# Where the values times their bonus are made: ScalarE instead of GpSimd, in a kernel of three stages

## The reference

```
def _attn_ref(r, k, v, w, u):                    # (batch 2, heads 8, seq 768, dim 48)
    state = zeros((B, H, D, D))
    for t in range(S):
        kt, vt, rt = k[:, :, t], v[:, :, t], r[:, :, t]
        cur = einsum('bhd,bhe->bhde', u[None] * kt, vt)
        y[:, :, t] = einsum('bhd,bhde->bhe', rt, state + cur)
        state = w[None, :, :, None] * state + einsum('bhd,bhe->bhde', kt, vt)
...
attn_out -> x (2, 768, 384) -> _moe_ref (8 experts, 384 -> 1024 -> 384) -> _moe2_ref (384 -> 1024, spatial 768 x 768, 512 -> 384)
```

## Time and profile before

| | |
|---|---|
| median of 3 runs | 408.51 us (406.87 to 411.73) |
| the profiled execution | 408.09 us, of which 405.9 us span |
| busy, share of the span | TensorE 375.8 us (93%), VectorE 195.7 (48%), ScalarE 141.1 (35%), GpSimd 188.0 (46%) |
| mean granted TensorE clock | 0.975 of full speed |

### The profile page before, as it was taken

The page is one execution under the profiler, slowest core; times in us unless marked ns, Lnnn a source line. Parts: engine busy times, 40 slices in busy tenths (PEclk is TensorE's granted clock), DMA queues, the critical chain, the costliest instruction groups (busy, mean ns, idle before and its releaser), DMA issues.

```text
span 405.9 us, 6203 instructions
## 1 busy us (share of the span) xinstructions
PE 375.8 (93%) x2523; PEld 354.3 (87%) x2523; DVE 195.7 (48%) x353; ACT 141.1 (35%) x215; POOL 188.0 (46%) x145
## 2 busy tenths in 40 slices
PE   5899999998689999979899999589999999999997
PEld 5799899886679998969799999547999998899996
DVE  7699889326692725262343522105505532803530
ACT  1022322212253736453444506006621224731122
POOL 2796899302938593949385607366500000510000
PEclk9899999879899999999999999979999999999999
DMA  7979979510195858776765710144000011000002
GB/s 237 412 253 376 378 286 366 202 41 19 29 346 171 289 174 295 234 233 209 258 225 164 251 73 28 40 119 116 2 0 2 0 58 60 2 0 2 0 19 97
DMA packets 30672, 61.58 MB, mean 152 GB/s; under 512 B 2418, under 2 KB 17651, under 8 KB 30643
## 3 DMA queue, kind: packets, MB, share of 16 engines
q1 hardware_dynamic: 23634, 47.80, 33.9%
q10 hardware_dynamic: 5216, 7.87, 5.4%
q0 software_dynamic: 1792, 5.51, 4.3%
HBM read 51.33 MB, written 9.83 MB: 151 GB/s over the span
## 4 chain that ended last, share of the span: by engine, by line
PE 58%; DMA 15%; POOL 15%; ACT 5%; issue 4%; DVE 3%; SPq 1%; DVEq 0%; POOLq 0%; ACTq 0%
POOL w_l L393 13%; PE bank L1225 12%; PE bank L1227 12%; PE bank L1226 12%; DMA x_in<-x_dram,inv 11%; PE bank L1152 5%; PE bank L1109 3%; POOL x_in L565 2%; PE bank L1148 2%; PE bank L1132 2%; PE bank L1098 2%; PE bank L1175 2%; DMA raw<-w_in 2%; ACT w_h L388 2%; DMA vN<-v_tok 2%
## 5 line engine op out<-in xcount | busy, mean ns | idle before, releaser
L393 POOL TENSOR_TENSOR w_l<-raw,w_h 128x1536 fp32r<-128x1536 f32 x24 | 87.0, 3637 | 36.6 <-ACT w_h L388 36.3
L1225 PE MATMUL bank<-xT_h,w_h 128*128 128x256 f32 x192 | 55.1, 287 | 2.1 <-DVE xT_l L780 2.1
L1226 PE MATMUL bank<-xT_l,w_h 128*128 128x256 f32 x192 | 55.0, 286 | 0.0
L1227 PE MATMUL bank<-xT_h,w_l 128*128 128x256 f32 x192 | 54.9, 286 | 0.0
L388 ACT ACTIVATE w_h<-raw 128x1536 fp32r<-128x1536 f32 x32 | 46.8, 1484 | 14.6 <-DVE inv L762 7.7
L604 POOL TENSOR_TENSOR v_l<-v_nrm,v_h 128x512 fp32r<-128x512 f32 x12 | 15.5, 1288 | 63.0 <-ACT v_h L1065 63.0
L1225 PE MATMUL bank<-w_h,hT_h 128*128 128x384 f32 x128 | 43.4, 339 | 0.0
L1227 PE MATMUL bank<-w_h,hT_l 128*128 128x384 f32 x128 | 42.8, 334 | 0.0
L1226 PE MATMUL bank<-w_l,hT_h 128*128 128x384 f32 x128 | 42.8, 334 | 0.0
L1009 ACT ACTIVATE hT_h<-bank 128x512 fp32r<-128x512 f32 x32 | 18.9, 594 | 60.4 <-PE bank L1227 60.4
L1225 PEld LDWEIGHTS bank<-xT_h,w_h 128*128 128x128 f32 x192 | 37.5, 196 | 2.3 <-DVE xT_l L780 2.3
(11 more groups left out here) (188 smaller groups left out, 840.3 us busy)
## 6 DMA issues: line engine op xcount, KB each, us to landing
raw<-w SPq DMA_DIRECT2D x28, 768.0 KB, 6.6
vN<-v_tok SPq DMA_DIRECT2D x6, 576.0 KB, 5.3
rT<-r_feat SPq DMA_DIRECT2D x6, 512.0 KB, 7.0
kT<-k_feat SPq DMA_DIRECT2D x6, 512.0 KB, 8.5
kN<-k_tok SPq DMA_DIRECT2D x6, 512.0 KB, 8.0
raw<-w ACTq DMA_DIRECT2D x4, 768.0 KB, 11.1
y_dram<-y_out SPq DMA_DIRECT2D x16, 192.0 KB, 1.9
rN<-r_tok SPq DMA_DIRECT2D x6, 384.0 KB, 6.6
```

The costliest lines, as they stand in the source:

```text
L393: eng.tensor_tensor(low, raw_of(n), high.bitcast(F32), ALU.subtract).then_inc(s_low[kind], 1)
L1225: mm(dst, left_h, right_h, start=(k == 0), stop=False)
L1226: mm(dst, left_h, right_l, start=False, stop=False)
L1227: return mm(dst, left_l, right_h, start=False, stop=(k == last_k))
```

## The change

GpSimd's two products of a chunk and its two waits go. ScalarE makes the same values in a new function `own_values(n)`, with eight instructions, one for each head: a copy of 48 values with a scale that is a pointer to that head's bonus of each token. It stands in ScalarE's loop ahead of `rowsT_of(n - 1)`, and behind the keys of chunk n+1. ScalarE now waits for the load of `vN` (at even n) and for s_bonus of the same chunk, and the last of the eight sets s_vc. The rest of both streams is as it was.

```diff
@@ gpsimd
             for n in range(NC):
-                p, q = divmod(n, 2)
                 if n + 2 < NC:
                     bonus_products(n + 2)
-                if q == 0:
-                    pool.wait_ge(s_slot_v[p % 2], 16 * (p // 2 + 1))
-                pool.wait_ge(s_bonus, n + 1)
-                for g in range(2):
-                    done = nc.gpsimd.tensor_tensor(X[:, n, :].rearrange("p (n g e) -> p n g e", n=NP, g=2)[:, :, g, :],
-                                                   vN[:, p % 2, q, :, g * 2 * DH:g * 2 * DH + DH],
-                                                   bonus[:, q * H + g:(q + 1) * H:2]
-                                                   .rearrange("p (n a) -> p n a", a=1)
-                                                   .to_broadcast([P, NP, DH]), ALU.mult)
-                done.then_inc(s_vc, 1)
                 if n == 1:
...
@@ scalar
+            def own_values(n):
+
+                p, q = divmod(n, 2)
+                if q == 0:
+                    act.wait_ge(s_slot_v[p % 2], 16 * (p // 2 + 1))
+                act.wait_ge(s_bonus, n + 1)
+                for h in range(H):
+                    m, g = divmod(h, 2)
+                    done = nc.scalar.activation(X[:, n, h * DH:(h + 1) * DH],
+                                                vN[:, p % 2, q, m, g * 2 * DH:g * 2 * DH + DH], ACT.Copy,
+                                                scale=bonus[:, q * H + h:q * H + h + 1])
+                done.then_inc(s_vc, 1)
+
             keys_of(0)
             for n in range(NC):
                 if n + 1 < NC and (n + 2) % NCB:
                     keys_of(n + 1)
+                own_values(n)
                 if n == NC - 1:
                     logit_of(n - 2)
                 if n:
                     rowsT_of(n - 1)
```

## The result

The changed kernel took 418.17 us (median of 4, 418.08 to 419.25), the kernel before 409.42 (406.87 to 411.73, 4 runs). The ratio is 1.0206, with a 95% interval of 1.0156 to 1.0256: slower by about 8.8 us, where 407.9 was forecast, with 404.5 to 412.0 as the range. The profiled execution took 418.16 us with a span of 416.4.

A forecast was written before the change was run, and what follows sets the result against it. The prediction took TensorE's pace to bound the attention stage, the only one changed. From the profiled 408.09 us, minus 0.21 for VectorE's relief and plus 0.06 for ScalarE's block gave 407.9, range 404.5 to 412.0.

The forecast's parts named there:

- What is removed: Prediction's part on GpSimd's dropped products (L521), 15.8 us: worth nothing by itself, with a second effect on VectorE.
- The splits at L393 inside the stage come a little earlier: GpSimd's weight splits in attention free raw buffers sooner, but the loads stand behind others in SP's order; costed at 0.
- VectorE's stretch: VectorE's L643 and L644 run 8.0 us over their best beside GpSimd; 2.4 us forecast to return, bounds 0 and 8.0.
- The minus 0.21 us: In chunk 1, L677 comes some 0.8 us earlier, removing TensorE's 0.21 us wait at its first transpose of X.
- ScalarE's block: Eight scaled copies a chunk on ScalarE: 333 ns each, holding the queue 1.80 us, bounds 0.6 and 2.67.
- its places: Where the block lies ahead of L957: it fits in most chunks, nothing at chunk 4, plus 0.06 us at chunk 6.
- The slower one: Rival: ScalarE's block misses chunk 4's deadline, stalls 2.0 us, and the clock falls, 3.4 more: 413.5 us; chance 0.12.
- The tail's fall of the clock: Half clock from 78.5 us, costing 3.4 us; expected to remain, with a rival that it stays away: 404.5, chance 0.12.
- VectorE's pace: Rival: VectorE's queue sets the attention stage's pace; gains 2.4 us, 405.7, or 8.0, 400.1; chance 0.08.

The follow-up runs named there:

- e6: Changed kernel with GpSimd waiting for the next chunk's bonus sum ahead of the second weight split (chunk 7) alone; 408.03 us, ratio to before 1.0076.
- e4: Kernel before, all work kept, with GpSimd's three weight splits moved ahead of its products of the same chunk; 416.12 us, ratio 1.0154.
- e5: The changed kernel run once more, unaltered; 415.07 us, ratio to the kernel before 1.0247.
- e2: Kernel before, GpSimd's products kept, with ScalarE's eight copies a chunk added into a spare buffer nobody reads; 411.30 us, ratio 0.9981.
- e9: Kernel before with GpSimd's three weight splits moved behind its last products of attention; 409.45 us, ratio 0.9945.
- e8: Changed kernel with GpSimd's three weight splits moved behind attention's last bonus sum; 408.70 us, ratio to before 1.0088.
- e10: Repeat of the changed kernel with GpSimd's extra bonus-sum wait ahead of all three weight splits; 411.73 us, ratio to before 1.0035.
- e3: Changed kernel with one 384-column copy without the bonus factor replacing ScalarE's eight; routing changed, 2715 matmuls instead of 2523; 489.32 us.
- e7: Changed kernel with one 384-column copy at a fixed factor of -0.02 replacing ScalarE's eight copies; 413.85 us, ratio to before 1.0155.
- e1: Changed kernel with GpSimd waiting for the next chunk's bonus sum ahead of each weight split in attention; 411.84 us, ratio to before 1.0029.

## Why the prediction was wrong

**The step that failed** is one sentence under "What is removed": "The splits at L393 inside the stage come a little earlier", costed at 0. I had followed what waits for the splits and not what they run beside. They did come earlier (41.52 and 53.84 against 45.28 and 56.76), from beside VectorE's masks to just ahead of two instructions that they hold. One wait of GpSimd gives back 7.0 us (e6), and moving the splits alone puts 9.01 and 10.19 us into the kernel before where it had 6.12 and 6.13 (e4). What it took to see it was in the trace of before: a split lasts 3.7 us, and VectorE's L643 and L644 stretch where a much shorter product of GpSimd runs beside them.

**VectorE's stretch** was forecast to shrink by 2.4 us. It grew: L632 has a mean of 1156 ns against 992, L633 949 against 1033.

```profile
L632 DVE TENSOR_TENSOR k_dec<-kT,tab_k 128x512 f32<-128x512 f32 x12 | 13.9, 1156 | 0.9 <-DMA kT<-k_feat 0.8
L633 DVE TENSOR_TENSOR r_dec<-rT,tab_r 128x512 f32<-128x512 f32 x12 | 11.4, 949 | 0.0
```

A share of GpSimd's time was the wrong measure; what counts is which instructions meet, and how long GpSimd's is. The Trainium skill, "SBUF — State Buffer", section "SBUF: two separate sides", has the rule that I cited for the relief alone: whoever starts first keeps the shared pair for the whole instruction and the other fully blocks. The traces agree with it here: k_dec started 0.15 us behind the split, ended 0.55 us behind the split's end at 44.95, and took 3.83 us, 3.15 over its 0.68: nearly all of it ran after the split, not beside it.

**The minus 0.21 us** did not come about. TensorE's wait at this place grew from 0.21 to 0.88 us (the first TensorE line above), and k_dec and r_dec ahead of it are as long as before: GpSimd's L506 and L509 ran beside them now. VectorE's timeline, then GpSimd's:

```profile
19.12 1.49 DVE L632 TENSOR_TENSOR k_dec<-kT,tab_k 128x512 f32<-128x512 f32 x1
20.53 1.48 DVE L633 TENSOR_TENSOR r_dec<-rT,tab_r 128x512 f32<-128x512 f32 x1
```
```profile
18.74 1.31 POOL L506 TENSOR_TENSOR rN<-rN,kN 128x384 f32<-128x384 f32 x1
20.14 1.33 POOL L509 TENSOR_TENSOR rN<-rN,u_bc 128x384 f32<-128x384 f32 x1
```

The first copy came 0.98 us earlier (23.12 against 24.10), but so did all of the chunk: state_sum started at 17.83 against 19.01. The same kernel has its first copy at 25.90 in e5, so the earlier start is no gain that can be credited to the change. The wait can be put down to it with more right: all eight traces without L521 have one for L666 in chunk 1 or 2, of 0.84 to 0.89 us in seven and 0.29 in e5, and the four traces with L521 have 0.21 (before), 0.51 (e2) and none (e4, e9). So this term looks like a small loss, by the mechanism of the failed step; no run isolates it.

**ScalarE's block** was right: 1.90 us for eight, 322 ns each, against 1.80 + 0.11 and 333 forecast. So were its places: chunk 4 cost nothing, and in chunk 6 the copy L946 came directly behind the block, 0.22 us late in the distance 4-5, without a wait of TensorE for it. With 5-6 the two distances are 11.49 in e2 and 11.35 in before, so this place cost 0.14 us, where 0.06 was forecast. e2 prices the copies at 0.9981 (0.9934 to 1.0028).

**The rivals.** The slower one, ScalarE missing its deadline, was the wrong mechanism with half of the right ending: a wait of TensorE (2.68 us, on VectorE) and then the clock, 3.2 us. The tail's fall of the clock came and went as said (8.90 in 9-10 before, 7.29 after, 5.67 in e8 and e10). VectorE's pace was a rival only as a gain; the same queue could lose time as well, and that case was missing from the range.

**Open.** Why the median moved by 8.8 us both times, when the two long distances give 6.0 and 5.2 us. In e5's trace inv is 6.9 us behind e6's: 4.7 of it are in 5-6 and 6-7, 2.0 at the start of the stage. From the last copy to inv it takes 13.2 us against 11.0 in the kernel before, at a clock of 0.50 between 90 and 100 us. No run ties the start or this fall to the change.

## What to carry to other kernels

When work is taken off an engine, list what it will now do earlier, and lay each long instruction of it beside the other engines' timelines at the new time; GpSimd's long operations with SBUF operands belong next to VectorE's PSUM work or to its idle time. An order that happens to fit is worth pinning with a semaphore wait: here one line was worth 7 us. A hold of 3.8 us cost 0.4 us at one place here and about 6 at another, by what is queued behind it and whether TensorE's clock falls.

## What the runs showed of the hardware

- VectorE's product of two SBUF operands, 0.68 us alone, took 3.8 to 3.9 us when it started 0.15 to 0.4 us behind GpSimd's product of 3.4 to 3.8 us. In e3 it started 1.22 us behind, took 2.76 us and ended 0.54 us behind the other's end, as elsewhere. The other way round, GpSimd's product took 3.89 us in place of 3.44 when it started 0.41 us behind VectorE's (before, at 56.76 and 68.42). VectorE's masks with one PSUM operand kept 1.27 us for two beside the same product.
- After a single wait of 1.89 to 2.81 us in a stretch where it was otherwise busy all the time, TensorE ran at 1.2 GHz in all five traces that have one. In the changed kernel, e5 and e7 the granted clock fell after the wait had ended and stayed there for 6.8 us (62.2 to 69.0 in the changed kernel); in e3 and e4 it fell before the wait ended and stayed for 10.2 us (58.1 to 68.3 in e4). Two waits of about 0.5 us did it in e8 and not in e1.
- The same code behind inv took 306.0 to 314.8 us in eleven traces, and 314.4 and 306.7 us in two traces of the same kernel.
